# Mixture of experts on one core: the transposes move from TensorE to DMA and VectorE, and the down product to two tiles behind the up product

## The chip, the core and the metric

The program runs on one core of a Trainium2 chip. The time is that of the device for one execution, in microseconds. The kernel before takes 1138.88 us (median of 3 runs, 1138.87 to 1140.42).

## The reference

The input is 3072 tokens (4 sequences of 768) of width 512, all fp32. Three parts follow each other: decayed linear attention (8 heads of 64), a mixture of 8 experts where each token goes to one, and a feed-forward network. The change is in the second:

```python
def _moe_ref(x, w_gate, w_output_gate, w1, w2):      # x 3072x512, w1 8x512x1024, w2 8x1024x512
    e_idx = np.argmax(x @ w_gate, axis=1)
    ...
    for e in range(E):
        mask = e_idx == e
        h = np.maximum(x[mask] @ w1[e], 0.0)
        ye = h @ w2[e]
        out[mask] = gate_w[mask, None] * eom[mask, e, None] * ye
```

The FFN after it is `g = h - tanh(h)` with `h = x @ w_in` (512 to 2048) and `g @ w_out`.

## The kernel before

Every product is split: an fp32 number is a high part (rounded to the type fp32r) and a low part, and three products (low by high, high by high, high by low, lines 1025 to 1027 in `split_product`) are summed in PSUM.

Attention works through 24 tiles of 128 tokens. GpSimd scatters each tile's rows to the DRAM tensor `x_sorted`, sorted by expert, and VectorE, from line 721 on, works out tables: for each of 31 expert tiles (`MOE_TILES`: 24 + 7) its first row, its weight slot and how many weight pieces must be ready.

The expert stage, on which the change bears, does for each tile i of 128 rows:
- `load_rows` (ScalarE's DMA queue, L511): the rows to `xs_sb`, 256 KB.
- `transpose_rows` (TensorE, L1032): four 128x128 products with the identity to PSUM bank 0. `x_hi` (ScalarE, L521) and `x_lo` (VectorE, L760) write high and low part to SBUF.
- `hidden` (TensorE): the up product, 2 x 4 x 3 = 24 products of 512 columns, to banks 1 and 2. `relu` (ScalarE, L527) brings each half to `hid`.
- `transpose_hidden` (TensorE, L1058): eight 128x128 transposes to banks 3 and 4, then `hid_hi` (ScalarE, L532) and `hid_lo` (VectorE, L798).
- `rows_out` (TensorE): the down product, 8 x 3 = 24 products of 512 columns, to bank 5. `copy_rows` (VectorE, L805) copies the bank to `ys_sb`, `store_rows` (ScalarE's queue, L516) stores it to `y_sorted`.

Every engine works its own list in order, and semaphores tie them. TensorE's list in the loop is:

```python
with pe.Fori(2, MOE_TILES) as i:
    hidden(i)
    transpose_rows(i + 1)
    pe.wait_ge(ys_copied, i - 1)
    rows_out(i - 1)
    transpose_hidden(i)
```

so the down product stands one tile behind the up product. Before the stage and around its start TensorE multiplies zeros (`stay_warm`) to keep its clock.

The weights lie in two slots in SBUF, for even and odd experts, as high and low part. SyncE loads them in pieces of 128x1024 (512 KB) to four buffers `raw`, and GpSimd splits each (`split_piece`: a tiny `gate` L365, the high part L379, the low part L383). A set has 8 pieces, the first four of w1, the last four of w2. `split_pieces` for expert e + 2 waits until the last down product of expert e is done (`ys_done`). After the eight experts come two more sets, `w_in` and `w_out`.

When all rows are stored, GpSimd gathers them back in token order (L396), VectorE scales them, and the FFN runs over 6 tiles of 512 tokens; its products are on lines 1126 to 1128 (up) and 1025 to 1027 (down), and VectorE works out the tanh between them (L850 to L873).

## Time and profile before

| | |
|---|---|
| median of 3 runs | 1138.88 us |
| the profiled execution, its own time | 1138.32 us |
| its span, first to last instruction | 1136.5 us |
| TensorE (PE) busy | 1087.8 us, 96% |
| VectorE (DVE) busy | 665.3 us, 59% |
| ScalarE (ACT) busy | 329.1 us, 29% |
| GpSimd (POOL) busy | 360.9 us, 32% |
| mean granted TensorE clock | 0.977 |
| moved by DMA | 107.25 MB, mean 94 GB/s |

The span is what the rows cover; 1.8 us lie around it. PE is TensorE's products, PEld its weight loads, which overlap them. A product is shown until its modelled end, so the distance between two starts tells its cost. The clock is a share of 2.4 GHz. The attention lies in the first 165 us, the expert stage from there to 565, the FFN from 580 to the end.

### The profile page before, as it was taken

The numbers are of one execution on the slowest core, as the hardware profiler recorded it, in microseconds if no ns is written. First come the engines' busy times: TensorE is split into PE (matmuls) and PEld (weight loads), VectorE is DVE, ScalarE is ACT, GpSimd is POOL, SyncE is SP. The second block draws the span as 40 slices with busy tenths as digits, with TensorE's granted clock in tenths as the row PEclk, the third lists the DMA queues.
The fourth block names the chain that finished last, engine by engine and source line by source line (L and its number), as shares of the span: only waits on it lengthen the run. The fifth ranks groups of instructions, "written<-read, shape, count | busy, mean of one in ns | idle before, by whom it ended". The sixth has DMA issues, their size and how long they took to land.

```text
span 1136.5 us, 18848 instructions
## 1 busy us (share of the span) xinstructions
PE 1087.8 (96%) x5953; PEld 907.2 (80%) x5954; DVE 665.3 (59%) x1175; ACT 329.1 (29%) x632; POOL 360.9 (32%) x316
## 2 busy tenths in 40 slices
PE   8978797999999999999978999999999999999998
PEld 7867686888888888888766887888888888888887
DVE  4888975212212222222159787877876887777775
ACT  2432321222222222222112333333333333333333
POOL 2454549193663874874094000000000000000000
PEclk9998998999999999999988999999999999999999
DMA  9975645152433443443140001000000000100101
GB/s 338 340 253 193 226 147 159 63 175 90 155 115 120 148 156 114 154 146 122 37 130 10 19 10 46 9 18 37 18 18 37 18 18 0 55 0 0 38 1 37
DMA packets 44223, 107.25 MB, mean 94 GB/s; under 512 B 5280, under 2 KB 5664, under 8 KB 44192
## 3 DMA queue, kind: packets, MB, share of 16 engines
q1 hardware_dynamic: 31280, 77.73, 19.9%
q10 hardware_dynamic: 9072, 16.52, 4.6%
q0 software_dynamic: 3840, 12.59, 3.4%
q8 instruction: 19, 0.31, 0.1%
q14 instruction: 12, 0.10, 0.0%
HBM read 84.01 MB, written 22.81 MB: 94 GB/s over the span
## 4 chain that ended last, share of the span: by engine, by line
PE 82%; DVE 11%; issue 3%; DMA 2%; ACT 1%; POOL 0%; SPq 0%; DVEq 0%; ACTq 0%; POOLq 0%
PE banks L1025 17%; PE banks L1027 17%; PE banks L1026 17%; PE banks L1126 7%; PE banks L1128 7%; PE banks L1127 7%; PE banks L1058 2%; DVE onehot L646 2%; PE banks L1032 1%; PE banks L945 1%; PE banks L933 1%; PE banks L926 1%; DVE q_scaled L668 1%; DVE probs L675 1%; PE banks L1105 1%
## 5 line engine op out<-in xcount | busy, mean ns | idle before, releaser
L383 POOL TENSOR_TENSOR w_sb<-raw,w_sb 128x1024 fp32r<-128x1024 f32 x80 | 192.5, 2407 | 6.7
L1126 PE MATMUL banks<-x2T_hi,w_sb 128*128 (+1 forms) x384 | 154.3, 402 | 7.2 <-DVE g_sb L868 7.2
L1128 PE MATMUL banks<-x2T_lo,w_sb 128*128 (+1 forms) x384 | 152.0, 396 | 0.0
L1127 PE MATMUL banks<-x2T_hi,w_sb 128*128 (+1 forms) x384 | 151.7, 395 | 0.0
L1025 PE MATMUL banks<-w_sb,g_lo 128*128 128x512 f32 x384 | 149.8, 390 | 0.0
L1026 PE MATMUL banks<-w_sb,g_hi 128*128 128x512 f32 x384 | 149.7, 390 | 0.0
L1027 PE MATMUL banks<-w_sb,g_hi 128*128 128x512 f32 x384 | 149.6, 390 | 0.0
L396 POOL DMA_INDIRECT gathered<-y_sorted,row_back x20 | 22.1, 1107 | 364.3 <-DVE x_sb L833 363.7
L760 DVE TENSOR_TENSOR xsT_lo<-banks,xsT_hi 128x512 fp32r<-128x512 f32 x32 | 22.1, 691 | 159.1 <-ACT xsT_hi L521 159.1
L577 ACT ACTIVATE square<-banks 128x512 f32<-128x512 f32 x96 | 57.4, 598 | 196.0 <-PE banks L1128 196.0
L584 ACT ACTIVATE g_hi<-g_sb 128x512 fp32r<-128x512 f32 x96 | 60.7, 632 | 169.5 <-PE banks L1027 151.6
L1025 PE MATMUL banks<-w_sb,xsT_lo 128*128 (+1 forms) x248 | 101.0, 407 | 7.3 <-DVE xsT_lo L760 7.3
L1025 PE MATMUL banks<-w_sb,hidT_lo 128*128 x248 | 99.9, 403 | 1.8 <-DVE hidT_lo L798 1.8
L873 DVE TENSOR_TENSOR g_lo<-g_sb,g_hi 128x512 fp32r<-128x512 f32 x96 | 69.0, 719 | 54.8 <-ACT g_hi L584 54.3
L805 DVE COPY ys_sb<-banks 128x512 f32<-128x512 f32 x31 | 21.4, 692 | 131.7 <-PE banks L1027 131.7
L1027 PE MATMUL banks<-w_sb,xsT_hi 128*128 (+1 forms) x248 | 98.2, 396 | 0.0
L1026 PE MATMUL banks<-w_sb,xsT_hi 128*128 (+1 forms) x248 | 97.6, 393 | 0.0
L1027 PE MATMUL banks<-w_sb,hidT_hi 128*128 x248 | 97.2, 392 | 0.0
L1026 PE MATMUL banks<-w_sb,hidT_hi 128*128 x248 | 96.7, 390 | 0.0
L1126 PEld LDWEIGHTS banks<-x2T_hi,w_sb 128*128 128x128 f32 x384 | 73.4, 191 | 22.9 <-issue 7.9
L1128 PEld LDWEIGHTS banks<-x2T_lo,w_sb 128*128 128x128 f32 x384 | 73.2, 191 | 15.8
L1127 PEld LDWEIGHTS banks<-x2T_hi,w_sb 128*128 128x128 f32 x384 | 73.5, 192 | 14.7
(137 smaller groups left out, 1914.4 us busy)
## 6 DMA issues: line engine op xcount, KB each, us to landing
raw<-in_weights SPq DMA_DIRECT2D x80, 512.0 KB, 3.4
xs_sb<-x_sorted ACTq DMA_DIRECT2D x32, 256.0 KB, 2.9
y_sorted<-ys_sb ACTq DMA_DIRECT2D x31, 256.0 KB, 2.1
kT_sb<-in_kT SPq DMA_DIRECT2D x24, 256.0 KB, 3.4
qT_sb<-in_qT SPq DMA_DIRECT2D x24, 256.0 KB, 4.1
kn_sb<-in_kn SPq DMA_DIRECT2D x24, 256.0 KB, 4.2
vn_sb<-in_vn SPq DMA_DIRECT2D x24, 256.0 KB, 4.8
out_rows<-out_sb SPq DMA_DIRECT2D x24, 256.0 KB, 2.2
```

Source lines behind the costliest of these rows:

```text
L383: nc.gpsimd.tensor_tensor(w_sb[:, s, 1, lo:hi], raw[:, p % RAW_SLOTS], w_sb[:, s, 0, lo:hi].bitcast(fp32), ALU.subtract).then_inc(piece_do ...
L577: nc.scalar.activation(square[:, c % 2], at(4 + c % 2), ACT.Square).then_inc(square_done, 1)
L584: nc.scalar.activation(g_hi[:, c % 2], g_sb[:, c % 2], ACT.Copy).then_inc(g_hi_done, 1)
L646: V.tensor_scalar(one(onehot, t), ranked[:, 0], route[:, 0:1], None, ALU.is_equal).then_inc(onehot_done, 1)
L873: V.tensor_tensor(g_lo[:, c % 2], g_sb[:, c % 2], g_hi[:, c % 2].bitcast(fp32), ALU.subtract)\
L1025: T.matmul(out_, lo, w_hi, start=first, stop=False)
L1026: T.matmul(out_, hi, w_hi, start=False, stop=False)
L1027: return T.matmul(out_, hi, w_lo, start=False, stop=last)
L1058: last = T.transpose(at(3 + n)[:, k * P:(k + 1) * P], hid[:, cols], ident[:])
L1126: T.matmul(out_, w_lo, hi, start=first, stop=False)
L1127: T.matmul(out_, w_hi, hi, start=False, stop=False)
L1128: return T.matmul(out_, w_hi, lo, start=False, stop=last)
```

## The change

- The row loads become four DMAs for each tile, one for each 32 partitions, with runs of 128 numbers (512 B), so that 32x32 block transposes on VectorE (`V.transpose`) give the transposed tile in SBUF, `xsT`.
- The hidden rows go through DRAM: after both relus ScalarE's queue stores `hid` to `hid_rows` (512 KB, runs of 1 KB) and loads it back as `hid_quads` (4 KB for each partition); VectorE's block transposes write `hidT`. `hid_hi` and `hid_lo` read `hidT` in SBUF, and their results have two buffers each. TensorE has no transposes left in this stage.
- `rows_out` stands two tiles behind `hidden`. The loop bodies hold two tiles.
- GpSimd splits the w1 half of a set when the last up product of that slot's expert is done, the w2 half when its last down product is. The first half of `w_out` is split before the gathers.
- The rows of w1 and w2 are put in the order that the block transposes give, on the host, where they were reordered before too.

Cut to its core, the diff is:

```diff
-MOE_BYTES = 24 * 1024
+MOE_BYTES = 40 * 1024
...
+    hid_rows = nc.dram_tensor("hid_rows", [QUADS, P, F_MOE // QUADS], fp32, kind="Internal").ap()
...
+    xs_sb = c_.place("xs_sb", [P, QUADS, D // QUADS])
+    xsT = c_.place("xsT", [P, DK, P])
...
+    hid_quads = c_.place("hid_quads", [P, QUADS, F_MOE // QUADS])
+    hidT = c_.place("hidT", [P, FK, P])
+    hidT_hi = c_.place("hidT_hi", [P, 2, FK, P], fp32r)
+    hidT_lo = c_.place("hidT_lo", [P, 2, FK, P], fp32r)
...
+            def split_pieces(m, s, before=None):
+                if before is not None:
+                    pool.wait_ge(hid_done, before * 2)
+                for p in range(W2_AT // PIECE):
+                    split_piece(m, s, p)
+                if before is not None:
+                    pool.wait_ge(ys_done, before)
+                for p in range(W2_AT // PIECE, SET_PIECES):
                     split_piece(m, s, p)
...
-            pool.wait_ge(ys_done, before)
-            split_pieces(EXPERTS // 2, 0)
+            split_pieces(EXPERTS // 2, 0, before)
+            pool.wait_ge(hid_done, 2 * MOE_TILES)
+            for p in range(W2_AT // PIECE):
+                split_piece(EXPERTS // 2, 1, p)
...
             pool.wait_ge(ys_done, MOE_TILES)
-            split_pieces(EXPERTS // 2, 1)
+            for p in range(W2_AT // PIECE, SET_PIECES):
+                split_piece(EXPERTS // 2, 1, p)
...
+                if first:
+                    row = 0
+                else:
+                    act.wait_ge(xsT_done, i)
+                    row = act.value_load(load_row[0:1, bass.ds(i, 1)], min_val=0, max_val=EXPERTS * REGION_ROWS - P)
+                rows = x_sorted[bass.ds(row, P)].rearrange("(g b) c -> b g c", g=QUADS)
+                for quad in range(QUADS):
+                    cols = slice(quad * (D // QUADS), (quad + 1) * (D // QUADS))
+                    act.dma_start(xs_sb[quad * QUAD:(quad + 1) * QUAD], rows[:, :, cols]).then_inc(xs_ready, 16)
...
+                nc.scalar.activation(xsT_hi[:].rearrange("p a n -> p (a n)"), xsT[:].rearrange("p a n -> p (a n)"), ACT.Copy)\
+                  .then_inc(xsT_hi_done, 1)
...
+            def store_hidden(i):
+                act.wait_ge(relu_done, i * 2 + 2)
+                act.dma_start(hid_rows.rearrange("i p f -> p i f"), hid[:].rearrange("p (i f) -> p i f", i=QUADS))\
+                   .then_inc(hid_stored, 16)
+            def load_hidden(i):
+                act.wait_ge(hid_stored, i * 16 + 16)
+                act.dma_start(hid_quads[:].rearrange("p g f -> p (g f)"), hid_rows.rearrange("i (b g) f -> (i b) (g f)", g=QUADS))\
+                   .then_inc(hid_ready, 16)
+            def hid_hi(i, number):
+                if number >= 2:
+                    act.wait_ge(ys_done, i - 1)
                 for n in range(2):
                     act.wait_ge(hidT_done, i * 2 + (n + 1))
-                    nc.scalar.activation(hidT_hi[:, n * DK:(n + 1) * DK].rearrange("p a n -> p (a n)"), at(3 + n), ACT.Copy)\
-                      .then_inc(hidT_hi_done, 1)
-
+                    cols = slice(n * DK, (n + 1) * DK)
+                    nc.scalar.activation(hidT_hi[:, number % 2, cols].rearrange("p a n -> p (a n)"),
+                                         hidT[:, cols].rearrange("p a n -> p (a n)"), ACT.Copy).then_inc(hidT_hi_done, 1)
...
+            def moe_step(i, number):
+                relu(i, 0)
+                if number >= 1:
+                    hid_hi(i - 1, number - 1)
+                if number >= 3:
+                    store_rows(i - 3)
+                relu(i, 1)
+                store_hidden(i)
+                if number + 1 < MOE_TILES:
+                    x_hi(i + 1)
+                load_hidden(i)
+                if number + 2 < MOE_TILES:
+                    load_rows(i + 2)
...
+            for i in range(3):
+                moe_step(i, i)
+            with act.Fori(3, MOE_TILES - 2, 2) as i:
+                moe_step(i, 3)
+                moe_step(i + 1, 4)
+            for i in (MOE_TILES - 2, MOE_TILES - 1):
+                moe_step(i, i)
+            hid_hi(MOE_TILES - 1, MOE_TILES - 1)
+            for i in range(MOE_TILES - 3, MOE_TILES):
                 store_rows(i)
...
+            def transpose_rows(i, first=False):
+                dve.wait_ge(xs_ready, i * (16 * QUADS) + 16 * QUADS)
+                if not first:
+                    dve.wait_ge(xsT_lo_done, i)
+                V.transpose(xsT[:].rearrange("p k (g b) -> p g k b", g=QUADS),
+                            xs_sb[:].rearrange("p g (k a) -> p g k a", k=DK)).then_inc(xsT_done, 1)
...
+                V.tensor_tensor(xsT_lo[:].rearrange("p a n -> p (a n)"), xsT[:].rearrange("p a n -> p (a n)"),
...
+            def transpose_hidden(i):
+                dve.wait_ge(hid_ready, i * 16 + 16)
+                dve.wait_ge(hidT_lo_done, i * 2)
+                for n in range(2):
+                    ks = slice(n * DK, (n + 1) * DK)
+                    V.transpose(hidT[:, ks].rearrange("p k (b g) -> p g k b", g=QUADS),
+                                hid_quads[:].rearrange("p g (k a) -> p g k a", k=FK)[:, :, ks]).then_inc(hidT_done, 1)
...
+                    V.tensor_tensor(hidT_lo[:, par, cols].rearrange("p a n -> p (a n)"),
+                                    hidT[:, cols].rearrange("p a n -> p (a n)"),
+                                    hidT_hi[:, par, cols].rearrange("p a n -> p (a n)").bitcast(fp32), ALU.subtract)\
...
+            def moe_step(i, number):
+                if number >= 3:
+                    if number >= 4:
+                        dve.wait_ge(ys_stored, i * 16 - 48)
+                    copy_rows(i - 3)
+                if number >= 1:
+                    transpose_hidden(i - 1)
+                if number + 1 < MOE_TILES:
+                    transpose_rows(i + 1)
+                if number >= 1:
+                    hid_lo(i - 1, (number - 1) % 2)
+                if number + 1 < MOE_TILES:
+                    x_lo(i + 1)
+            for i in range(5):
+                moe_step(i, i)
+            with dve.Fori(5, MOE_TILES - 2, 2) as i:
+                moe_step(i, 5)
+                moe_step(i + 1, 6)
+            for i in (MOE_TILES - 2, MOE_TILES - 1):
+                moe_step(i, i)
+            last = MOE_TILES - 1
+            transpose_hidden(last)
+            hid_lo(last, last % 2)
+            for i in range(last - 2, last + 1):
+                dve.wait_ge(ys_stored, 16 * i)
+                copy_rows(i)
...
+                if not first:
+                    pe.wait_ge(relu_done, i * 2)
...
+            def rows_out(i, number, par):
...
+                if number >= 3:
+                    pe.wait_ge(ys_copied, i)
...
+                    last = split_product(at(5), hidT_hi[:, par, k], hidT_lo[:, par, k],
...
+            def moe_step(i, number):
                 hidden(i)
-                transpose_rows(i + 1)
-
-                pe.wait_ge(ys_copied, i - 1)
-                rows_out(i - 1)
-                transpose_hidden(i)
-            pe.wait_ge(ys_copied, MOE_TILES - 1)
-            rows_out(MOE_TILES - 1)
+                rows_out(i - 2, number, number % 2)
+            for i in range(2, 5):
+                moe_step(i, i)
+            with pe.Fori(5, MOE_TILES - 2, 2) as i:
+                moe_step(i, 5)
+                moe_step(i + 1, 6)
+            for i in (MOE_TILES - 2, MOE_TILES - 1, MOE_TILES):
+                if i < MOE_TILES:
+                    hidden(i)
+                rows_out(i - 2, i, i % 2)
+            rows_out(MOE_TILES - 1, MOE_TILES + 1, (MOE_TILES - 1) % 2)
...
-    w1 = moe_w1.reshape(EXPERTS, DK, P, F_MOE // WIDE, WIDE).transpose(0, 2, 3, 1, 4).reshape(EXPERTS, P, -1)
-    w2 = moe_w2.reshape(EXPERTS, FK, P, D).transpose(0, 2, 1, 3).reshape(EXPERTS, P, -1)
+    w1 = moe_w1.reshape(EXPERTS, QUADS, DK, QUAD, F_MOE // WIDE, WIDE).transpose(0, 1, 3, 4, 2, 5).reshape(EXPERTS, P, -1)
+    w2 = moe_w2.reshape(EXPERTS, QUADS, FK, QUAD, D).transpose(0, 1, 3, 2, 4).reshape(EXPERTS, P, -1)
```

The order of instructions, at three places. First ScalarE in its loop over tiles, one tile (L numbers are each kernel's own). Before:

```order
L527 ACTIVATE hid<-banks 128x512 [waits hid_done]
L521 ACTIVATE xsT_hi<-banks 128x512 [waits xsT_done]
...
L511 DMA xs_sb<-x_sorted 128x512
L532 ACTIVATE hidT_hi<-banks 128x512 [waits hidT_done] x2
L516 ISA [waits ys_copied]
L516 DMA y_sorted<-ys_sb 128x512
```

And in the change:

```order
L570 ACTIVATE hid<-banks 128x512 [waits hid_done]
L564 ACTIVATE hidT_hi<-hidT 128x512 [waits hidT_done,ys_done]
L564 ACTIVATE hidT_hi<-hidT 128x512 [waits hidT_done]
L539 ISA [waits ys_copied]
L539 DMA y_sorted<-ys_sb 128x512
L569 REGISTER_ALU
L570 ACTIVATE hid<-banks 128x512 [waits hid_done]
L549 DMA hid_rows<-hid 128x4x256 [waits relu_done]
L543 REGISTER_ALU
L544 ACTIVATE xsT_hi<-xsT 128x512 [waits xsT_done]
L553 ISA
L554 DMA hid_quads<-hid_rows 128x1024 [waits hid_stored]
```

The copies of the hidden rows, of the tile before now, stand between the two relus, `xsT_hi` behind the store's issue; the load waits in the list for the store, and the four row loads follow it.

Then VectorE in its loop, one tile. Before:

```order
L760 TENSOR_TENSOR xsT_lo<-banks,xsT_hi 128x512 [waits xsT_hi_done]
L815 ISA
L805 COPY ys_sb<-banks 128x512 [waits ys_done,ys_stored]
L796 ISA
L798 TENSOR_TENSOR hidT_lo<-banks,hidT_hi 128x512 [waits hidT_hi_done]
```

And in the change:

```order
L869 COPY ys_sb<-banks 128x512 [waits ys_done,ys_stored]
L849 REGISTER_ALU
L851 REGISTER_ALU [waits hid_ready]
L854 STREAM_TRANSPOSE hidT<-hid_quads 128x4x128 [waits hidT_lo_done]
L854 STREAM_TRANSPOSE hidT<-hid_quads 128x4x128
L804 ISA
L808 STREAM_TRANSPOSE xsT<-xs_sb 128x4x4x32 [waits xsT_lo_done,xs_ready]
L859 REGISTER_ALU
L861 TENSOR_TENSOR hidT_lo<-hidT,hidT_hi 128x512 [waits hidT_hi_done]
L859 REGISTER_ALU
L861 TENSOR_TENSOR hidT_lo<-hidT,hidT_hi 128x512 [waits hidT_hi_done]
L812 REGISTER_ALU
```

`xsT_lo` of the next tile is now last (it follows the last row shown), behind three transposes and two subtractions whose inputs both lie in SBUF.

Third, VectorE's last rows of this stage in the change:

```order
L854 STREAM_TRANSPOSE hidT<-hid_quads 128x4x128 [waits hidT_lo_done,hid_ready]
L854 STREAM_TRANSPOSE hidT<-hid_quads 128x4x128
L861 TENSOR_TENSOR hidT_lo<-hidT,hidT_hi 128x512 [waits hidT_hi_done] x2
L869 COPY ys_sb<-banks 128x512 [waits ys_done,ys_stored] x3
```

The copies for tiles 28, 29 and 30 stand behind the work on tile 30's hidden rows; before, only one copy did.

## Rows read from the trace of the kernel before

**Rows 1.** Stretches: busy us and instructions (x) per engine, then clock, DMA share, GB/s.
```profile
core 0: us, PE busy (x) PEld busy (x) DVE busy (x) ACT busy (x) POOL busy (x), PEclk, DMA share, GB/s
206.00:545.00 339.00, 339.00 (x1659) 282.30 (x1658) 73.67 (x111) 76.61 (x139) 199.43 (x168) 1.00 0.39 129
178.00:185.00 7.00, 0.00 (x0) 0.00 (x0) 6.72 (x11) 1.09 (x2) 6.83 (x7) 0.70 0.56 154
185.00:191.00 6.00, 5.80 (x14) 4.55 (x15) 1.15 (x2) 0.28 (x1) 5.92 (x6) 0.50 0.42 153
576.00:609.00 33.00, 24.64 (x93) 20.44 (x94) 25.61 (x22) 5.58 (x10) 31.38 (x24) 0.74 0.23 76
610.00:1136.00 526.00, 519.97 (x2325) 428.66 (x2324) 406.45 (x692) 181.77 (x324) 19.87 (x18) 1.00 0.07 21
```

**Rows 2.** Timeline of one step: start and duration in us, engine, line, operation.
```profile
445.05 0.39 PE L1027 MATMUL banks<-w_sb,hidT_hi 128*128 x1
445.28 1.03 PE L1058 MATMUL banks<-ident,hid 128*128 128x128 f32 x8
446.07 0.47 PE L1025 MATMUL banks<-w_sb,xsT_lo 128*128 x1
...
451.41 0.39 PE L1027 MATMUL banks<-w_sb,xsT_hi 128*128 x1
451.64 0.60 PE L1032 MATMUL banks<-ident,xs_sb 128*128 128x128 f32 x4
451.84 0.60 ACT L527 ACTIVATE hid<-banks 128x512 f32<-128x512 f32 x1 [2.12 <-PE banks L1027]
451.99 0.48 PE L1025 MATMUL banks<-w_sb,hidT_lo 128*128 x1
...
452.33 0.59 ACT L521 ACTIVATE xsT_hi<-banks 128x512 fp32r<-128x512 f32 x1
```

**Rows 3.** DMA issues from 200 to 550 us: count, size, median us to landing.
```profile
raw<-in_weights SPq DMA_DIRECT2D x56, 512.0 KB, 3.4
y_sorted<-ys_sb ACTq DMA_DIRECT2D x29, 256.0 KB, 2.1
xs_sb<-x_sorted ACTq DMA_DIRECT2D x28, 256.0 KB, 2.9
```

**Rows 4.** Groups by line, 200 to 550 us: busy us, mean ns, idle before.
```profile
L383 POOL TENSOR_TENSOR w_sb<-raw,w_sb 128x1024 fp32r<-128x1024 f32 x56 | 134.0, 2394 | 4.7
L379 POOL TENSOR_SCALAR w_sb<-raw 128x1024 fp32r<-128x1024 f32 x56 | 58.9, 1052 | 0.0
L798 DVE TENSOR_TENSOR hidT_lo<-banks,hidT_hi 128x512 fp32r<-128x512 f32 x58 | 37.4, 686 | 8.9 <-ACT hidT_hi L532 8.9
L805 DVE COPY ys_sb<-banks 128x512 f32<-128x512 f32 x29 | 20.1, 692 | 121.4 <-PE banks L1027 121.4
L365 POOL TENSOR_TENSOR gate_out<-gate_in 128x1 f32<-128x1 f32 x56 | 10.9, 194 | 122.1 <-PE banks L1027 122.1
```

**Rows 5.** Groups of VectorE at the FFN's start, 586 to 609 us.
```profile
L851 DVE TENSOR_SCALAR far<-square 128x512 uint8<-128x512 f32 x3 | 5.6, 1866 | 0.0
L853 DVE TENSOR_TENSOR tanh_sb<-tanh_sb,square 128x512 f32<-128x512 f32 x3 | 4.5, 1506 | 0.1
```

**Rows 6.** Timeline of GpSimd: the first instruction of two sets' splits.
```profile
457.89 0.19 POOL L365 TENSOR_TENSOR gate_out<-gate_in 128x1 f32<-128x1 f32 x1 [19.96 <-PE banks L1027]
...
494.69 0.19 POOL L365 TENSOR_TENSOR gate_out<-gate_in 128x1 f32<-128x1 f32 x1 [7.63 <-PE banks L1027]
```

**Rows 7.** Timeline of TensorE, the first product of up product 1.
```profile
185.20 0.79 PE L1025 MATMUL banks<-w_sb,xsT_lo 128*128 x1 [7.35 <-DVE xsT_lo L760]
```

**Rows 8.** Timeline of TensorE: last down product of the experts, and two FFN up products.
```profile
558.74 0.49 PE L1025 MATMUL banks<-w_sb,hidT_lo 128*128 x1 [1.78 <-DVE hidT_lo L798]
...
592.62 0.47 PE L1126 MATMUL banks<-x2T_hi,w_sb 128*128 128x512 f32 x1 [3.69 <-DVE g_sb L868]
...
601.48 0.79 PE L1126 MATMUL banks<-x2T_hi,w_sb 128*128 x1 [3.16 <-DVE g_sb L868]
```

More of the change, by code:

```diff
@@ new lines, in relu @@
+            def relu(i, n):
+                act.wait_ge(hid_done, i * 2 + (n + 1))
+                nc.scalar.activation(hid[:, n * WIDE:(n + 1) * WIDE], at(1 + n), ACT.Relu).then_inc(relu_done, 1)
+            def moe_step(i, number):
[11 more added lines that the diff above has]
+                    load_rows(i + 2)
@@ L1027, in split_product @@
                 return T.matmul(out_, hi, w_lo, start=False, stop=last)
-            def transpose_rows(i):
-                pe.wait_ge(xs_ready, i * 16 + 16)
-                for k in range(DK):
-                    last = T.transpose(at(0)[:, k * P:(k + 1) * P], xs_sb[:, k * P:(k + 1) * P], ident[:])
-                last.then_inc(xsT_done, 1)
             def hidden(i, first=False):
@@ L1074, in _ @@
             stay_warm(WARM_TAIL[2], still)
-            transpose_rows(0)
             stay_warm(WARM_TAIL[3], still)
```

68 lines of the change are left out of this document (7 added, 61 removed).

## The prediction

> **What bounds the kernel now.** I read the stretches first [rows 1]. Between 206 and 545 us PE is busy for all 339 us at full clock, so the expert stage is bound by PE's instruction stream: what leaves PE there leaves the time, as long as nothing becomes later than PE. VectorE is busy 22% of that stretch, ScalarE 23%, DMA 0.39. The other two places with losses are its start (178 to 185: PE does nothing) and the start of the last FFN (576 to 609: clock 0.74, VectorE and GpSimd both busy); from 610 on PE is full.
>
> Then the timeline of one step [rows 2]. The eight transposes of the hidden rows take the space from 445.28 to 446.07, 0.79 us, the four of the next input rows that from 451.64 to 451.99, 0.35 us. The rest of a step is 48 products, 24 in each block: the block from 446.07 to 451.64 is 5.57 us. So a step is 2 x 5.57 + 1.14 = 12.28 us.
>
> **The change part by part.** My sum is against the profiled execution, 1138.3 us (span 1136.5); the median of the runs is 1138.9.
>
> *a) Transposes leave PE.* 31 steps x 1.14 = **35.3 us less**, if PE stays the bound with a step of 11.14 us. PE's register loads at a block's head now follow a product and not transposes. I give them nothing: at the same place before FFN blocks PE shows no hole (520 of 526 us busy [rows 1]). Bounds: 0 and 0.1 us at each of 62 heads.
>
> *b) The hidden rows' new path* must fit its place. Call 0 the end of up product i. ScalarE's relu starts 0.2 later (451.84 against 451.64) and takes 0.5; then come a 512 KB store, a 512 KB load behind it, two VectorE transposes, two ScalarE copies, two VectorE subtractions. For the store the nearest rows are 2.1 us (256 KB store) and 3.4 (512 KB load), for the load 2.9 and 3.4, with 3.4 the likelier for both sizes [rows 3]; I take 2.9 + 3.5 = 6.4. A transpose is on no row. Its nearest rows are 128x512 operations with one input: 0.69 us for a copy out of PSUM [rows 4], and 1.87 for an SBUF operation beside GpSimd [rows 5]. I take 0.7, because it has one input and is in no fast form, and keep 1.87 for the range. By the Trainium skill ("SBUF — State Buffer", Who interferes with whom) an operation with one SBUF input outside the two-port modes doesn't meet GpSimd; no row here shows that for a transpose.
> So rows are back at about 7.4 us, transposed at 8.9, and ScalarE, after the next tile's first relu at 8.5 to 9.1, finishes its two copies at 10.4. The down product of that tile starts four blocks later, at 22.3: ten us to spare. There is a tighter loop: ScalarE's relu of i+1 comes behind these copies in its queue. Relu 0.6 + store and load 6.4 + transpose 0.7 + copies 1.2 + y store and gaps 0.7 = 9.6 us, against a step of 11.14. Store plus load may grow from 6.4 to about 7.9 before this loop sets the step.
>
> *c) VectorE meets GpSimd.* Its three subtractions per tile now have both inputs in SBUF. With one input in PSUM, 58 of them took 0.686 us although GpSimd was splitting for 199 of the 339 us [rows 1, 4]; at the FFN's start the SBUF form took 1.51 beside the same splits [rows 5]. So each costs up to 0.8 more on average, at worst the 2.39 us of GpSimd's long instruction. The order on VectorE is then: transposes to 9.6, hidden subtractions to about 13, then x_lo of the next tile. That last one can't start before ScalarE's x_hi, which is now behind the issue of the store: 0.85 + 0.36 + 0.65 gives 1.9 after the end of up product i+1, that is 13.0. It ends at 14.6, at worst 16.3, and PE needs it at 16.7 (one block after 11.14). The cover is thin but there. I book **3 us** for the steps in which several waits fall together (bounds 0 and 20, the latter 0.65 in each step).
>
> *d) Weights.* A half set is four pieces of 0.19 + 1.05 + 2.39 = 3.64, or 14.6 us [rows 4]; slowed by VectorE perhaps 16.6. The first half starts when the last up product has read the slot, the second 27 us later (five blocks). The shortest expert has three tiles: its releases lie 36.8 apart, three old steps [rows 6], 33.4 now. Two halves are 29 to 33 us, the next expert of four tiles gives 44.6, and GpSimd idled 122 us in this stage. I count nothing; PE would pay only if splits came to 4.2 us apiece.
>
> *e) Start.* Up product 1 waits, as before (7.35 us at 185.20 [rows 7]), for x_lo(1) behind the routing arithmetic. That arithmetic begins after x_lo(0), which now needs four smaller loads, a transpose and a wait for GpSimd's running split: +1.8. The transpose and copy of tile 1 used to be over long before; now they stand behind the arithmetic: +1.4, and the subtraction may wait, +1.1. So **+4.3**. Then up product 2 follows without a down product between them, so relu 0.8, store issue 0.36, x_hi 0.65 and x_lo 0.8 lie open: **+2.7**.
>
> *f) End.* VectorE's list ends: transpose and subtract tile 30, and only then copy the sums of tile 28. PE's down product 29 waits for that copy, its one bank. Up product 30 ends at 0, down product 28 at 5.6, the subtractions of tile 30 at about 12.1 (GpSimd is splitting again), the copy at 12.9: **7.3 us of nothing on PE**, where 1.8 were lost before [rows 8]. Before, 7 idle us took the clock down, and 5.8 us with 14 products ran at 0.50 [rows 1]: 0.42 each instead of 0.23, **+2.6**. Down product 30 directly behind 29 lays open one copy, **+0.95**. Also this drain is one down product longer, which only moves that block from the start: no cost. Together +9.1.
>
> *g) FFN start.* GpSimd has four pieces of the last set split during f), so it is in VectorE's way until about 27 us after the last down product and not until 44. The first tanh chain still meets it, the second and third don't. PE's waits of 3.69 and 3.16 us there, and the low clock behind them [rows 1, 8], shrink by **5.5 us** (bounds 2 and 9).
>
> Sum: -35.3 + 3 + 4.3 + 2.7 + 9.1 - 5.5 = -21.7, so **1116.6 us**. About 0.2%, 2.3 us, is what a measurement of this kernel can tell from no change.
>
> **The rivals.**
> *R1, the round trip becomes the bound and the kernel slower.* Place: the loop of b). While GpSimd splits, a 512 KB piece is loaded each 3.6 us beside 1.5 MB per step of row traffic instead of 0.5; the landing times of [rows 3] come from queues half empty (DMA share 0.39). The result is slower once the average step passes 11.14 + 21.7/31 + 0.1 = 11.94, that is store plus load 8.7 us and more in all steps, or 7.9 with transposes of 1.5. With 10 us for the two the loop is 13.2: 29 x 2.1 more, some 1177 us. Against it: loads keep 4 KB rows, stores 1 KB, and in a third of the time no weights are loaded. The Trainium skill ("VectorE: DVE Perf Modes", The three transpose paths) warns that a plain DMA transposing by strides is 19 times slower than the transposing DMA when the innermost stride is large; it would apply to single elements, and here whole runs of 512 B or 1 KB are moved. Chance 0.11.
> *R2, the cover of c) is too thin.* VectorE's waits, or a transpose of 1.2 to 1.9 us, make x_lo late by 0.3 to 0.6 us in most steps while GpSimd works: +8 to +16, 1122 to 1135 us, 1127 the middle. For it: three locks in 11 us, each up to 2.39. Against: in the FFN's start two and a half such operations fitted in every split. Chance 0.22.
> *R3, the edges cost less.* The end's wait doesn't lower the clock, the start's subtractions meet no split, g) gives 9: -35.3 + 5 + 5 - 9 = -34, 1104 us. Chance 0.15.
> *R4, PE gains nothing from a)*, because PE was held by something else in the steps (an output bank, a register load): 1138 plus e) and f), within 0.2% if g) cancels them. Nothing in [rows 1] shows a hold. Chance 0.02.
>
> **The numbers.** The forecast's own case has 0.50. Faster: 0.50 + 0.22 + 0.15, less 0.02 for R2's end = 0.85; same 0.04 (R4 and the borders of R1, R2); slower 0.11. The range runs from just under R3 to the end of R2, 1101 to 1135; R1 above it and a little below are left out.
>
> **What would show it.** Right: PE in the expert stage without a hole and products in a step of 11.1 us; no instruction on PE with identity and hidden rows; hidden load landing near 3.5 us; VectorE's two-input subtractions at 1.2 to 1.6 us while GpSimd splits, about 0.7 otherwise; one hole of some 7 us before the next to last down product, ended by VectorE's copy of sums; an idle GpSimd between the half sets. Wrong: PE waiting on x_lo in most steps (R2), or ScalarE's relu starting well after the product it waits for, with the load of the hidden rows as what ended the wait of VectorE's transpose (R1); PE waiting for GpSimd's splits would refute d).

## The result, and the profile after

The changed kernel takes 1129.91 us (median of 12 runs, 1123.8 to 1136.16) where the kernel before takes 1138.86 (12 runs, 1136.35 to 1140.42): a ratio of 0.9919, 95% interval 0.9901 to 0.9936. It is faster by 9 us, and I had forecast 22. Its runs lie 12 us apart, those of before 4. The profiled execution took 1125.78 us (span 1124.0).

The transposes did leave PE. What came in their place is on the page; first its busy times, then its DMA issues (KB each, median us from issue to landing):

```profile
PE 1047.3 (93%) x5577; PEld 866.1 (77%) x5578; DVE 784.1 (70%) x1267; ACT 337.6 (30%) x631; POOL 382.6 (34%) x316
```
```profile
raw<-in_weights SPq DMA_DIRECT2D x80, 512.0 KB, 4.0
hid_rows<-hid ACTq DMA_DIRECT2D x31, 512.0 KB, 4.1
hid_quads<-hid_rows ACTq DMA_DIRECT2D x31, 512.0 KB, 4.4
```

Stretches of the changed kernel (us, then busy us of PE, its weight loads, VectorE, ScalarE and GpSimd, each with its count, granted clock, DMA share, GB/s):

```profile
200.00:520.00 320.00, 304.30 (x1317) 246.88 (x1316) 186.26 (x191) 84.17 (x137) 219.58 (x168) 0.99 0.73 228
440.00:480.00 40.00, 40.00 (x178) 32.97 (x177) 24.41 (x25) 10.06 (x17) 28.77 (x22) 1.00 0.73 231
```

Before, PE was busy in every microsecond of the expert stage [rows 1]. Now it idles 15.7 of the 320 us from 200 to 520, at a DMA share of 0.73 where it had been 0.39 [rows 1]. From 440 to 480 it is full, so a step without a hole is there too; two starts of an up product in it:

```profile
434.08 0.39 PE L1104 MATMUL banks<-w_sb,xsT_lo 128*128 x1
...
444.96 0.39 PE L1104 MATMUL banks<-w_sb,xsT_lo 128*128 x1
```

Such a step takes 10.88 us, and not the 11.14 that I had worked out from the kernel before: 24 products take 5.44 us here, where the same 24 behind a group of transposes had taken 5.57. Over the 28 steps between the first down product and that of tile 28 this can be held against what was measured:

```profile
204.06 0.39 PE L1104 MATMUL banks<-w_sb,hidT_lo 128*128 x1
...
530.30 0.39 PE L1104 MATMUL banks<-w_sb,hidT_lo 128*128 x1
```

They took 326.2 us, 11.65 each, where 28 times 10.88 is 304.6: the steps lose 21.6 us. Of these 15.6 are holes, and 6.0 are slower products behind the holes: behind a wait of about 1.2 us the 24 products took 5.55 to 5.58 us, and behind the longest one, 3.11 us at 421.45, they took 7.19 at a granted clock of 0.76 (421 to 428 us). The groups of 200 to 520 on PE say in front of which product the idle time lies (last figure: idle us before the group, and what ended them):

```profile
L1104 PE MATMUL banks<-w_sb,xsT_lo 128*128 x222 | 89.2, 402 | 15.7 <-DVE xsT_lo L813 13.7 <-issue 1.9
...
L1104 PE MATMUL banks<-w_sb,hidT_lo 128*128 x217 | 84.4, 389 | 0.0
```

The idle time is always in front of an up product, waiting for VectorE's low part of the input rows; the down products, two tiles behind, never wait. It looks as if VectorE were late (my term c). But VectorE's own groups of 200 to 540 have it waiting elsewhere:

```profile
L861 DVE TENSOR_TENSOR hidT_lo<-hidT,hidT_hi 128x512 fp32r<-128x512 f32 x58 | 76.5, 1358 | 0.0
L854 DVE STREAM_TRANSPOSE hidT<-hid_quads 128x512 f32<-128x512 f32 x59 | 60.0, 1094 | 112.8 <-DMA hid_quads<-hid_rows 112.8
L813 DVE TENSOR_TENSOR xsT_lo<-xsT,xsT_hi 128x512 fp32r<-128x512 f32 x28 | 28.5, 1019 | 6.2 <-ACT xsT_hi L544 6.2
L808 DVE STREAM_TRANSPOSE xsT<-xs_sb 128x512 f32<-128x512 f32 x28 | 19.4, 693 | 10.7 <-DMA xs_sb<-x_sorted 10.7
```

VectorE idles 112.8 us for the hidden rows' load. The chain of waits of the stretch 240 to 270 goes through that load without ever touching PE (start us, us, what):

```profile
by line: DMA hid_quads<-hid_rows 42.9%; DMA hid_rows<-hid 40.3%; DVE hidT L854 8.2%; issue 7.2%; ACT hid L570 6.1%; ACTq L539 2.7%; ACT hidT_hi L564 0.3%; DVEq L851 0.3%; ACTq L569 0.2%; DVEq L807 0.1%
...
250.09 0.61 ACT hid L570
...
250.72 4.48 DMA hid_rows<-hid
...
255.21 5.10 DMA hid_quads<-hid_rows
...
260.43 0.13 DVE hidT L854
...
261.37 1.11 DVE hidT L854
...
262.50 0.06 ACT hidT_hi L564
...
263.14 0.61 ACT hid L570
```

That is the loop of my part b): second relu, store, load, both transposes, ScalarE's copy, the next second relu. One turn takes 263.14 - 250.09 = 13.05 us: 0.61 + 4.48 + 5.10, then 2.2 for the two transposes, and 0.66 to the relu. The turn before, with landings of 3.15 and 3.89, took 10.5. So the loop is store + load + 3.45 us, and with the page's medians (4.1 and 4.4) it is 11.95, longer than PE's step of 10.88. It isn't one turn alone: the 28 turns from the second relu at 206.57 to the one at 531.93 took 9.7 to 13.7 us, 11.62 on average, close to the 11.65 of PE's steps; in 23 of them the second relu did not wait for PE at all. ScalarE's timeline shows what hangs on it (start us, us, instruction, idle before and releaser):

```profile
255.21 0.33 ACTq L554 DMA_DIRECT2D hid_quads<-hid_rows  x1
...
259.44 0.60 ACT L570 ACTIVATE hid<-banks 128x512 f32<-128x512 f32 x1 [7.35 <-PE banks L1106]
261.57 0.63 ACT L564 ACTIVATE hidT_hi<-hidT 128x512 fp32r<-128x512 f32 x1 [1.53 <-DVE hidT L854]
262.50 0.63 ACT L564 ACTIVATE hidT_hi<-hidT 128x512 fp32r<-128x512 f32 x1 [0.30 <-DVE hidT L854]
...
263.14 0.60 ACT L570 ACTIVATE hid<-banks 128x512 f32<-128x512 f32 x1
...
264.28 0.63 ACT L544 ACTIVATE xsT_hi<-xsT 128x512 fp32r<-128x512 f32 x1 [0.54 <-ACT hid L570]
```

Between the two relus of a tile ScalarE waits for the hidden rows of the tile before. Behind the second relu stands x_hi (L544) of the next input, on which x_lo and PE wait. The second relu at 263.14 has no idle time before it and no release by PE: its product was done.

The two ends, on PE's timeline:

```profile
187.14 0.79 PE L1104 MATMUL banks<-w_sb,xsT_lo 128*128 x1 [8.09 <-DVE xsT_lo L813]
196.92 0.79 PE L1104 MATMUL banks<-w_sb,xsT_lo 128*128 x1 [2.71 <-DVE xsT_lo L813]
...
256.39 0.49 PE L1104 MATMUL banks<-w_sb,xsT_lo 128*128 x1 [1.24 <-DVE xsT_lo L813]
...
544.17 0.79 PE L1104 MATMUL banks<-w_sb,hidT_lo 128*128 x1 [8.27 <-issue]
...
545.18 0.63 PE L1106 MATMUL banks<-w_sb,hidT_hi 128*128 x1
545.61 0.63 PE L1104 MATMUL banks<-w_sb,hidT_lo 128*128 x1
...
552.92 0.49 PE L1104 MATMUL banks<-w_sb,hidT_lo 128*128 x1 [1.02 <-issue]
...
558.49 7.75 PE L1084 MATMUL banks<-ident 128*128 128x128 f32 x68
```

"issue" at 544.17 names no releaser; VectorE's timeline does. The copy of the sums of tile 28, whose bank down product 29 needs, stands behind all work on tile 30's hidden rows and ends at 543.95:

```profile
539.36 2.02 DVE L854 STREAM_TRANSPOSE hidT<-hid_quads 128x512 f32<-128x512 f32 x2 [4.27 <-DMA hid_quads<-hid_rows]
541.24 2.11 DVE L861 TENSOR_TENSOR hidT_lo<-hidT,hidT_hi 128x512 fp32r<-128x512 f32 x2
543.27 0.68 DVE L869 COPY ys_sb<-banks 128x512 f32<-128x512 f32 x1
```

### The profile page after: what moved, and what is told of

It is laid out like the page before. It is cut to its first block, busy times and chain, and to the rows that moved or that the text cites. A ratio compares the mean times of both kernels' runs of the same rounds, so it can differ in the third digit from the quotient of the medians.

```text
span 1124.0 us, 18489 instructions
## 1 busy us (share of the span) xinstructions
PE 1047.3 (93%) x5577; PEld 866.1 (77%) x5578; DVE 784.1 (70%) x1267; ACT 337.6 (30%) x631; POOL 382.6 (34%) x316
## 4 chain that ended last, share of the span: by engine, by line
PE 59%; DMA 17%; DVE 13%; issue 6%; ACT 2%; ACTq 1%; POOL 1%; DVEq 0%; SPq 0%; POOLq 0%
PE banks L1104 11%; PE banks L1106 10%; PE banks L1105 10%; DMA hid_quads<-hid_rows 7%; PE banks L1196 7%; PE banks L1198 7%; PE banks L1197 7%; DMA hid_rows<-hid 7%; DVE onehot L691 2%; DVE hidT L854 2%; DMA vn_sb<-in_vn 1%; PE banks L1005 1%; ACT hid L570 1%; PE banks L1012 1%; DVE q_scaled L713 1%
## 5 line engine op out<-in xcount | busy, mean ns | idle before, releaser
L397 POOL TENSOR_TENSOR w_sb<-raw,w_sb 128x1024 fp32r<-128x1024 f32 x80 | 198.3, 2479 | 6.7
L854 DVE STREAM_TRANSPOSE hidT<-hid_quads 128x512 f32<-128x512 f32 x62 | 63.0, 1094 | 115.0 <-DMA hid_quads<-hid_rows 115.0
L1104 PE MATMUL banks<-w_sb,hidT_lo 128*128 x248 | 97.6, 394 | 9.3 <-issue 9.3
L952 DVE TENSOR_TENSOR g_lo<-g_sb,g_hi 128x512 fp32r<-128x512 f32 x96 | 66.5, 693 | 54.1 <-ACT g_hi L629 53.6
L570 ACT ACTIVATE hid<-banks 128x512 f32<-128x512 f32 x62 | 37.1, 598 | 195.9 <-PE banks L1106 145.5
L393 POOL TENSOR_SCALAR w_sb<-raw 128x1024 fp32r<-128x1024 f32 x80 | 91.9, 1149 | 0.0
L1196 PEld LDWEIGHTS banks<-x2T_hi,w_sb 128*128 128x128 f32 x384 | 72.8, 190 | 20.1 <-issue 5.7
L1198 PEld LDWEIGHTS banks<-x2T_lo,w_sb 128*128 128x128 f32 x384 | 72.6, 189 | 15.6
```

The costliest lines, as they stand in the source:

```text
L393: nc.gpsimd.tensor_scalar(w_sb[:, s, 0, lo:hi], raw[:, p % RAW_SLOTS], 1.0, 1.0, ALU.mult, ALU.mult)\
L397: nc.gpsimd.tensor_tensor(w_sb[:, s, 1, lo:hi], raw[:, p % RAW_SLOTS], w_sb[:, s, 0, lo:hi].bitcast(fp32), ALU.subtract).then_inc(piece_do ...
L854: V.transpose(hidT[:, ks].rearrange("p k (b g) -> p g k b", g=QUADS), hid_quads[:].rearrange("p g (k a) -> p g k a", k=FK)[:, :, ks]).then ...
L952: V.tensor_tensor(g_lo[:, c % 2], g_sb[:, c % 2], g_hi[:, c % 2].bitcast(fp32), ALU.subtract)\
L1104: T.matmul(out_, lo, w_hi, start=first, stop=False)
L1196: T.matmul(out_, w_lo, hi, start=first, stop=False)
```

## The experiments

Three theories for the holes in the steps. **L**: the loop just shown, so that landing times and transposes set the step. **G**: VectorE's subtractions with both inputs in SBUF are held by GpSimd (term c). **Q**: the order on VectorE alone, with the hidden rows' subtractions ahead of x_lo. All runs stand against the kernel before, timed beside them (medians 1137.63, 1139.66 and 1138.19 us in three sets). Set 1 holds the first four below, set 2 the next four, set 3 the last three. The changed kernel, timed again in set 1, gave 0.9946 against its 0.9919 of before; so what a kernel of sets 2 and 3 gains over the changed one is given from both. A table behind the last run says where in each profile the time went.

**The changed kernel again** (as_changed, no edit). 

> The change again, unaltered, as the measure for the runs beside it. Its profile showed 15.7 us of holes on TensorE between 200 and 520 us, nearly all ended by VectorE's x_lo, one hole of 8.3 us before down product 29 and slow products behind it. All theories expect some 1130 us (1124 to 1136) and 10 to 20 us of holes; since the store and the load of the hidden rows land after 4.1 and 4.4 us instead of the 2.9 and 3.5 that I had taken, and these times vary, I expect the spread of the runs to come from there.

Measured 1131.15 us (1127.31 to 1134.21), 0.9946 [0.9932, 0.996]. PE idles 15.5 us of 200 to 520, as in the first profile.

**copy_before_last**: the copy and store of tile 28's sums ahead of the last tile's transposes.
```
+ dve.wait_ge(ys_stored, 16 * (last - 2))
+ copy_rows(last - 2)
  transpose_hidden(last)
...
+ store_rows(MOE_TILES - 3)
  hid_hi(MOE_TILES - 1, MOE_TILES - 1)
```


> Only the end of the expert stage differs: VectorE copies the sums of tile 28 before it turns to the hidden rows of tile 30, and ScalarE's list stores them before its last copies. If the 8.3 us hole is that queue order and the slow products behind it are its consequence: the hole before down product 29 goes, a shorter one of 1 to 3 us may stand before down product 30, no product at 0.43 us, together 8 to 10 us less than as_changed. If down product 29 waits for its operands: nothing changes (within 1 us).

Measured 1120.2 us, 0.9838 [0.9802, 0.9875], 11 to 12 less than the changed kernel beside it, though its six runs lie 14 us apart. PE's timeline has no 8.27 us any more, but two waits of 1.02 in front of the last two down products, of which this is the second:

```profile
547.36 0.49 PE L1107 MATMUL banks<-w_sb,hidT_lo 128*128 x1 [1.02 <-DVE ys_sb L870]
```

So part f) holds in mechanism and place, and in price by the profiles: from the start of down product 28 to the end of the last one it is 18.9 us instead of 27.7 to 28.2, 9 less, while the steps lose what they lost before.

**xlo_first**: x_lo ahead of the hidden rows' subtractions on VectorE.
```
- if number >= 1:
-     hid_lo(i - 1, (number - 1) % 2)
  if number + 1 < MOE_TILES:
      x_lo(i + 1)
+ if number >= 1:
+     hid_lo(i - 1, (number - 1) % 2)
```


> VectorE's order in each step: x_lo of the next tile before the two hidden subtractions, instead of behind them. Theory Q (the queue): TensorE's holes come from x_lo standing behind two subtractions that each may wait for GpSimd, while its own operand is ready; then nearly all of the 15.7 us of holes between 200 and 520 go, 10 to 15 us less than as_changed. Theory L (the loop): ScalarE's relu comes late because the hidden rows' round trip through DRAM is longer than a step allows; then the order changes little, 0 to 3 us.

Measured 1130.92 us, 0.9945 [0.9926, 0.9964]: nothing. VectorE's groups of 200 to 540 say why:

```profile
L813 DVE TENSOR_TENSOR xsT_lo<-xsT,xsT_hi 128x512 fp32r<-128x512 f32 x29 | 37.6, 1296 | 44.6 <-ACT xsT_hi L544 44.6
```

x_lo now waits 44.6 us for x_hi instead of 6.2. VectorE reaches it earlier, ScalarE doesn't. Q falls, and what is late stands before ScalarE's x_hi.

**lo_from_psum**: the subtractions' first operand read from PSUM.
```
- V.tensor_tensor(xsT_lo[:]..., xsT[:]..., xsT_hi[:]..., ALU.subtract)
+ V.tensor_tensor(xsT_lo[:]..., at(0), xsT_hi[:]..., ALU.subtract)
...
- hidT[:, cols].rearrange("p a n -> p (a n)"),
+ at(3 + n),
```


> The three subtractions of a tile read their first operand from PSUM banks 0, 3 and 4 (old contents, nobody writes them in this stage) instead of from SBUF: the low parts are not those of the rows, everything else is in place. Theory G (GpSimd's lock): with one input in PSUM they take 0.69 us each instead of 1.36 and 1.02, GpSimd's pieces are no longer slowed, and the holes shrink by more than half: 8 to 13 us less than as_changed. Theory L (the loop): the round trip is untouched, the holes stay, 0 to 4 us less.

Measured 1121.04 us, 0.9856 [0.9838, 0.9874], 10 less, between what the two theories gave it. The subtractions fell to half, yet PE still idles 12.7 us:

```profile
L861 DVE TENSOR_TENSOR hidT_lo<-banks,hidT_hi 128x512 fp32r<-128x512 f32 x60 | 37.8, 668 | 0.4 <-ACT hidT_hi L564 0.4
```
```profile
200.00:520.00 320.00, 307.29 (x1333) 249.44 (x1332) 143.50 (x195) 86.35 (x140) 200.05 (x168) 1.00 0.72 230
```

G is real and worth about 10 us, but the holes are not its alone. In its profile the 28 steps lose 17.2 us, 4 to 5 less than in the two profiles of the changed kernel (about 3 of it is less idle time, the rest faster products at clock 1.00 instead of 0.98 to 0.99), and the end is 1.4 to 2 us shorter. The whole span is 5.4 to 6.9 us shorter; the rest of the 10 lies between the profiled and the median executions and isn't placed.

**no_store**: the store and the wait for it are gone.
```
- act.dma_start(hid_rows.rearrange("i p f -> p i f"), ...).then_inc(hid_stored, 16)
- act.wait_ge(hid_stored, i * 16 + 16)
- act.dma_start(hid_quads[:]..., hid_rows.rearrange("i (b g) f -> (i b) (g f)", g=QUADS))
+ act.dma_start(hid_quads[:]..., tile_of(weights, 0))
```


> The store of the hidden rows is left out, and the load, issued at the same place, reads 512 KB of the weights instead (so it need not wait): the down products work on other numbers. The round trip is shorter by the store's 4.1 us, and 0.5 MB per step less are moved; the subtractions with both inputs in SBUF stay as they are. Theory L (the loop through DRAM sets the holes, GpSimd's lock only adds to it): hardly a hole between 200 and 520 us, 13 to 18 us less than the change, 1112 to 1118. Theory G (the lock makes VectorE late whatever the rows do): at least a third of the holes stays, 0 to 8 us less.

Measured 1103.39 us, 0.9684 [0.9667, 0.9701]: 27 to 30 less than the changed kernel, where 13 to 18 had been expected, about the holes alone. VectorE's transposes hardly wait, and PE is nearly full although the subtractions still take 1.19:

```profile
L858 DVE TENSOR_TENSOR hidT_lo<-hidT,hidT_hi 128x512 fp32r<-128x512 f32 x60 | 68.9, 1188 | 17.9 <-ACT hidT_hi L561 17.8
L851 DVE STREAM_TRANSPOSE hidT<-hid_quads 128x512 f32<-128x512 f32 x60 | 60.3, 1082 | 6.7 <-DMA hid_quads<-in_weights 6.6
```
```profile
200.00:520.00 320.00, 318.19 (x1392) 262.82 (x1391) 193.14 (x203) 83.73 (x146) 231.22 (x174) 0.99 0.58 188
```

L holds: with the store out of the loop the holes of the steps go, G's slow subtractions still there. Its 28 steps take 304.64 us, 10.88 each, so the 21.6 us are gone to the last. The run doesn't separate the store's time from its traffic (DMA share 0.58 instead of 0.73); both left with it. Another 4.8 us are the end, whose hole is 3.9 us here.

**store_halves**: each half of the hidden rows stored behind its own relu, into two buffers.
```
  relu(i, 0)
+ store_hidden(i, 0, number % 2)
...
  relu(i, 1)
- store_hidden(i)
+ store_hidden(i, 1, number % 2)
```


> The store is split: the first 256 KB leave as soon as the first relu is done, the second behind the second relu; hid_rows has two buffers for it. Outcome complete and in place. Theory L: what is left behind the second relu lands after some 2.5 to 3 us instead of 4.1, the loop is shorter by 1.2 to 1.6 us less the 0.4 of one more issue, the holes between 200 and 520 us shrink to under 8 us: 5 to 10 us less than the change. Theory G: 0 to 2 us less.

Measured 1123.61 us, 0.9866 [0.9847, 0.9884], 6 to 9 less; 11.3 us idle in 200 to 520, where I had expected under 8. The half behind the second relu was no quick store: the 256 KB stores landed after a median of 3.3 us, not 2.5 to 3. So the loop was cut by less than I had expected.

**even_transposes**: of the two transposes' output patterns, the hidden rows' is now the one without a step.
```
- V.transpose(hidT[:, ks].rearrange("p k (b g) -> p g k b", g=QUADS), ...)
+ V.transpose(hidT[:, ks].rearrange("p k (g b) -> p g k b", g=QUADS), ...)
...
- V.transpose(xsT[:].rearrange("p k (g b) -> p g k b", g=QUADS), ...)
+ V.transpose(xsT[:].rearrange("p k (b g) -> p g k b", g=QUADS), ...)
```


> The two transposes of the hidden rows write runs of 32 numbers (as the one of the input rows does, 0.69 us) and the one of the input rows writes with a step of four (as theirs do, 1.09 us); the rows keep their places in the end. If the pattern of the output sets the duration: 0.69 us for the hidden ones, 1.09 for the input's, and theory L then gives 0.8 us less in the loop, 2 to 6 us less than the change; if the duration hangs on something else, the lengths stay as they are and nothing moves.

Measured 1123.38 us, 0.9861 [0.984, 0.9881], 7 to 10 less. That is more than the 2 to 6 expected; in its profile the 28 steps lose 5.5 us less. The two durations changed places, so 0.8 us left each turn of the loop:

```profile
L854 DVE STREAM_TRANSPOSE hidT<-hid_quads 128x512 f32<-128x512 f32 x60 | 39.2, 690 | 113.8 <-DMA hid_quads<-hid_rows 113.8
L808 DVE STREAM_TRANSPOSE xsT<-xs_sb 128x512 f32<-128x512 f32 x28 | 30.9, 1102 | 21.1 <-DMA xs_sb<-x_sorted 20.9
```

**weights_only**: the kernel before with the weight halves split as their slots come free, and nothing else.
```
+ if before is not None:
+     pool.wait_ge(hid_done, before * 2)
+ for p in range(W2_AT // PIECE):
+     split_piece(m, s, p)
+ if before is not None:
+     pool.wait_ge(ys_done, before)
- for p in range(SET_PIECES):
+ for p in range(W2_AT // PIECE, SET_PIECES):
      split_piece(m, s, p)
```


> The kernel before with one part of the change alone: GpSimd splits the w1 half of a set when the last up product of its slot is done and the w2 half when the last down product is, and the first half of w_out before the gathers. TensorE had no wait for weights, so the expert stage stays at 12.3 us per step; term g) of the prediction says that the FFN's start gets shorter since GpSimd is out of VectorE's way sooner: 3 to 7 us less than before. The rival: the gathers start later because GpSimd is still splitting when the last row is stored (14.6 us of pieces against about 10 us from the last up product's end to the store's landing), 4 to 5 us of it given back: 0 to 3 us less.

Measured 1134.51 us, 0.9958 [0.9943, 0.9972], about 5 less than the kernel before: g)'s share, and it comes without the rest of the change. From the end of the last down product its profile takes 1127.4 - 559.33 = 568.1 us, where before took 572.2. The profiled execution is the fastest of its nine, 5.4 us under their median, so the 4.1 between these two is a single sample.

**relus_first**: both relus, the store and x_hi ahead of everything in ScalarE's list that waits for the hidden rows' load; for this `hid_rows` has two buffers. x_lo goes first on VectorE, which alone gave nothing.
```
  relu(i, 0)
+ relu(i, 1)
+ store_hidden(i, number % 2)
+ if number + 1 < MOE_TILES:
+     x_hi(i + 1)
  if number >= 1:
      hid_hi(i - 1, (number - 1) % 2)
...
      store_rows(i - 3)
- relu(i, 1)
- store_hidden(i)
- if number + 1 < MOE_TILES:
-     x_hi(i + 1)
- load_hidden(i)
+ load_hidden(i, number % 2)
```


> ScalarE's list in each step: both relus, the store and x_hi first, and only then the two copies of the tile before and its y store, then the load. hid_rows has two buffers, and VectorE takes x_lo before the hidden subtractions (alone that order changed nothing). So no relu waits for the round trip of the tile before, and the rows still have two tiles of time. Theory L: the loop is cut, the holes between 200 and 520 us go nearly all (under 4 us), 10 to 16 us less than the change, 1114 to 1120; the end's hole of 8 us stays. If the landing times themselves hold TensorE up, whatever the order: 0 to 4 us less.

Measured 1111.57 us (1109.06 to 1115.08), 0.9765 [0.9745, 0.9785]: 18 to 21 less than the changed kernel, with no transfer or instruction fewer, and more than the 10 to 16 expected. ScalarE's timeline:

```profile
284.02 0.60 ACT L570 ACTIVATE hid<-banks 128x512 f32<-128x512 f32 x1 [5.34 <-PE banks L1106]
286.74 0.60 ACT L570 ACTIVATE hid<-banks 128x512 f32<-128x512 f32 x1 [2.12 <-PE banks L1106]
287.37 0.40 ACTq L549 DMA_DIRECT2D hid_rows<-hid  x1
287.88 0.63 ACT L544 ACTIVATE xsT_hi<-xsT 128x512 fp32r<-128x512 f32 x1 [0.55 <-ACT hid L570]
```
```profile
200.00:520.00 320.00, 315.27 (x1371) 258.64 (x1372) 188.75 (x201) 81.46 (x143) 219.50 (x171) 0.99 0.75 234
```

Both relus now follow PE; the load landed in a median of 4.7 us here, no faster than before, and it no longer matters. PE is busy for 315.3 of 320 us. From 209.78 us on each second relu waits for PE, as the theory asks, and the 28 steps lose 5.3 us instead of 21.6. This is the run that settles L: same traffic, same transposes, same subtractions, only the order cut. The subtractions took 98 us in all from 200 to 520 (0.95 us for the hidden rows, 1.57 for x_lo), against 99 in the changed kernel. Two of its parts were not tested apart: x_lo first, which gave nothing in the old order, and the second buffer. The profiled span is 10.7 to 12.2 us shorter than the changed kernel's; the gain of 18 to 21 is that of the medians, since the changed kernel's was profiled in one of its faster executions and this one in its slowest.

**all_four**: store_halves, even_transposes and copy_before_last together, ScalarE's order in the steps kept (the diffs of the three above).
```
  relu(i, 0)
+ store_hidden(i, 0, number % 2)
...
+ V.transpose(hidT[:, ks].rearrange("p k (g b) -> p g k b", g=QUADS), ...)
...
+ copy_rows(last - 2)
  transpose_hidden(last)
```


> The change with three of its costs taken down and its list order kept: store in halves (alone -7), even transposes (alone -7), the end's copy ahead (alone -11). Theory L: the loop is shorter by some 2 us and falls under the step of 11.1 us, the holes in the steps nearly vanish; sum -20 to -25 against the change, 1106 to 1111 us. If the parts overlap: -15 to -18.

Measured 1112.58 us, 0.9775 [0.9755, 0.9796]: 16 to 19 less, where the three apart add up to 24 and more. But the holes did not nearly vanish: PE idles 10.2 us here, and the 28 steps still lose 14.3, where the halves alone left 17.0 and the transposes alone 16.1. Some turns are still long; behind one of them stands a load of the hidden rows of 7.2 us (from 245.2). The end gives 9 us, as it did alone. Taking time off the loop helps less than taking the wait out of the list.

**relus_first_all**: the same three edits, and the order of relus_first.
```
  relu(i, 0)
+ store_hidden(i, 0, number % 2)
+ relu(i, 1)
+ store_hidden(i, 1, number % 2)
+ if number + 1 < MOE_TILES:
+     x_hi(i + 1)
```


> The same, with the store in two halves, the even transposes and the copy of sums ahead of the last tile's work. Theory L: no holes left to shorten in the steps, so only the end's 9 to 11 us come on top of relus_first: 1104 to 1110 us, 29 to 35 below before. If every part still counts, it goes below 1104.

Measured **1100.3 us** (1098.51 to 1102.83), 0.9663 [0.9647, 0.9679]. This complete kernel beats both: 38 us less than before, and its runs are 4 us apart again. Against all_four, timed beside it, it differs in the order of the lists alone, and that is worth 12.3 us. Its stretch, and its first down product and that of tile 28:

```profile
200.00:520.00 320.00, 316.18 (x1384) 261.56 (x1385) 187.04 (x202) 84.77 (x148) 226.04 (x173) 0.99 0.75 237
```
```profile
211.94 0.39 PE L1109 MATMUL banks<-w_sb,hidT_lo 128*128 x1
...
516.58 0.39 PE L1109 MATMUL banks<-w_sb,hidT_lo 128*128 x1
```

That is 304.64 us for 28 steps, 10.88 each: nothing is lost in the steps any more. The 3.8 us that PE still idles in this stretch are at its start.

Where the time goes in each profile, from starts of products on PE's timeline. "Steps" is the time of the 28 steps above 304.6 us; "end" the time from the start of down product 28 to the end of the last one, above the 16.3 us of its 72 products:

| run | steps, us lost | end, us lost |
|---|---|---|
| the changed kernel, first profile | 21.6 | 11.9 |
| as_changed | 22.4 | 11.3 |
| copy_before_last | 22.7 | 2.6 |
| xlo_first | 20.0 | 11.3 |
| lo_from_psum | 17.2 | 9.9 |
| no_store | 0.0 | 7.1 |
| store_halves | 17.0 | 10.4 |
| even_transposes | 16.1 | 10.9 |
| relus_first | 5.3 | 11.9 |
| all_four | 14.3 | 2.7 |
| relus_first_all | 0.0 | 2.6 |

## Why the prediction was right or wrong

The sign and the range held, the size did not, and two errors of opposite sign met in it: the transposes were worth some 7 us more than I had booked, and the steps lost 18.6 us more. That the result stayed inside the range is luck: without the first error the second would have carried it past 1135. The two profiled spans differ by 12.5 us, the medians by 9; the ledger below is of the spans. The other 3.5 are the median runs of the changed kernel being 4 us over its profiled one. That the spread of the runs comes from varying landings in the loop is not shown: in relus_first_all, where the loop costs nothing, the runs lie 4 us apart, but in store_halves, whose steps still lose 17.0 us, the four runs lie within 1.6, and none of the longer executions of the changed kernel was profiled.

- *a) -35.3: right in kind, too small.* No product with identity and hidden rows is left in the steps, and from 440 to 480 PE has no hole. But the step without transposes is 10.88 us, not 11.14: 28 steps in a row take 304.64 us in no_store and in relus_first_all. I had taken the 5.57 us of a block for its products alone; it held 0.13 us that the switch from transposes to products cost, twice in each step. So the transposes were worth 12.29 - 10.88 = 1.41 us a step, 31 times that is 43.7, and the trace of before could have told it: inside a block, from 546.81 to 549.75 us, the products start 0.226 us apart, 24 of them 5.43.
- *b) the step that failed.* Store 2.9 taken, 4.1 measured; load 3.5, measured 4.4; transposes 0.7, measured 1.09, and both stand in the loop where I had counted one. I had drawn the right loop and its limit ("store plus load may grow to about 7.9"; by the trace it is 10.88 - 3.45 = 7.4). But I took the landing times from [rows 3], where the queues were half empty, and saw the rise from 0.39 to 0.73 in DMA share only as a rival's argument. They came to 8.5, so the loop was longer than PE's step on average, and 23 of 28 turns went by it. I had written that 3.4 us was the likelier for both sizes and then took 2.9 for the store; but 3.4 for both would still have lain under the limit. No row of before shows a landing at the load that the change creates.
- *c) +3 booked, 21.6 us lost in the 28 steps*, of which 15.6 are idle time: 18.6 more than booked. The miss of 9.2 us in the spans is this, plus 1.1 at the two ends, less the 10.6 by which a), e) up to up product 1, and g) came out better. The step named the victim rightly (x_lo, with a cover of 2 us) and the culprit wrongly. The lock is there (1.36 and 1.02 us for the subtractions, and lo_from_psum gives 10 us back). But relus_first gives 18 to 21 with subtractions that take as long in sum (98 us against 99 from 200 to 520), because what was late was ScalarE's x_hi behind a transfer. The cover and the loop were treated as two separate matters; they share ScalarE's list. The outcome falls into R2's range by R1's mechanism, and both signs that I had named for being wrong are there: PE waits for x_lo, in about half of the steps, and ScalarE's second relu starts behind the load of the hidden rows, in 23 of 28. R1 as I priced it, in every step and above the time before, did not happen, since turns of 10.5 us with quick landings stood among those of 13.05.
- *d) 0: nearly right.* Behind one single weight load of PE stood a wait of 2.5 us for a split; the step's products show none in front of the down products.
- *e) +4.3 and +2.7.* Up product 1 begins at 187.14 against 185.20 [rows 7]: +1.9. But the same point lies between 187.1 and 192.5 us in the profiles of the other versions with this start, and at 181.4 in weights_only, whose start is that of before: the stretch ahead varies by some us on its own, so this term is tested no better than that. The second is 2.71 in the trace, right.
- *f) +9.1: right.* A hole of 8.27 for 7.3; some ten products mostly 0.43 apart instead of 0.23, 2.0 for 2.6; 1.02 for 0.95; less the 1.78 of [rows 8]: 9.5. And its named cause carried the cheapest repair: moving one copy took 9 us off the end in the profile, and 11 off the median.
- *g) -5.5: right.* From the end of the last down product to the end of the span it is 1124.0 - 558.49 = 565.5 us against 572.2: -6.7, of which weights_only's profile, one fast execution, shows 4.1.

In sum: to up product 1 +1.9 (for +4.3); from there to the end of the last down product -7.8 (for -20.5, that is -35.3 + 3 + 2.7 + 9.1); from there on -6.7 (for -5.5). The middle part is some -42.3 for the transposes (the part of a) that lies behind up product 1), +21.6 for the steps, +2.8 for the start and +10.1 for the end. So the steps missed by 18.6 us, a) by 7 the other way, and all other terms by 2.4 or less.

The rule of the Trainium skill that I drew on ("SBUF — State Buffer", Who interferes with whom) did well on the transposes: the input rows' took 693 ns while GpSimd split for 219.6 of 320 us, like the copy out of PSUM of the same shape (692, [rows 4]), and the hidden rows' 1.09 came from their output pattern, as even_transposes shows. The loss of which the other rule (The three transpose paths) warns did not appear here: the strided store and load landed in about the time of a plain weight piece, 4.1 and 4.4 against 4.0.

## What to carry to other kernels

Before a detour through DRAM enters a kernel, write down the closed loop it makes through the in-order list of the engine that issues it, and put everything another engine waits for ahead of the first instruction that waits for the landing: with the same traffic this was 18 to 21 us of 1130. Price work that leaves the bound engine by the distance between undisturbed products, and not by the block next to it, which may carry part of its cost: here that was 0.26 us a step. A hole costs more than its length: behind 15.6 us of holes stood 6.0 us of slower products. Price transfers at the load the change itself creates, not at that of the profile before. When a wait on the bound engine names a producer, follow that producer's own idle time before shortening its work; xlo_first moved the named producer and gained nothing.

## What the hardware showed that I had not expected

- A VectorE transpose of 128x512 f32 in 32x32 blocks took 0.69 us with output in unbroken runs of 32 and 1.09 to 1.10 with a step of four elements, for either tensor (even_transposes swapped them).
- A 512 KB load of the hidden rows landed in 4.4 us at a DMA share of 0.73, and a load of the same size in 3.4 at 0.58 (no_store, where the source was a weight tile, so place and load are not separated). The landing of the same transfer varied from run to run: the 512 KB store of the hidden rows took a median of 4.1 us in the changed kernel and 3.2 in relus_first, its 256 KB half 3.3 in store_halves and 2.6 in relus_first_all.
- In the changed kernel a hidden-row subtraction with both inputs in SBUF took 1.36 us on average beside GpSimd's splits, 0.67 with one input in PSUM (lo_from_psum); in other orders it was 0.95 (relus_first) to 1.36. VectorE weighed on GpSimd too: in lo_from_psum its long split took 2398 ns, in the changed kernel 2497.
